# State product in 32-column tiles of the TensorE array, its PSUM banks moved next to the first-layer banks

## The reference

```python
# gated linear attention, 4 sequences of 768 tokens, 8 heads of 48
for t in range(S):
    state = alpha[:, :, t, :, None] * state + einsum('bhd,bhe->bhde', k[:, :, t], v[:, :, t])
    y[:, :, t] = einsum('bhd,bhde->bhe', q[:, :, t], state)
# four experts, 384 -> 1024 -> 384, weighted by normalised probabilities
h = np.maximum(x @ w1[e], 0.0);  out += p[:, e:e + 1] * (h @ w2[e])
# gated feed-forward, 384 -> 2048 -> 384
h = x @ w_in;  g = h * clip(h + 3, 0, 6) / 6;  out = g @ w_out
```

## Time and profile before

| | us |
|---|---|
| median of 3 runs | 1381.57 (1380.89 to 1384.29) |
| profiled execution, its own time | 1382.56 |
| span of the profiled execution, first to last instruction | 1380.6 |
| PE busy | 1356.1 (98%) |
| POOL, DVE, ACT busy | 790.9, 699.7, 534.8 |
| L438 matmuls (state product) | 704 records, 20.4 us busy |

### The profile page before, as it was taken

The page is one execution under the profiler, slowest core; times in us unless marked ns, Lnnn a source line. Parts: engine busy times, 40 slices in busy tenths (PEclk is TensorE's granted clock), DMA queues, the critical chain, the costliest instruction groups (busy, mean ns, idle before and its releaser), DMA issues.

```text
span 1380.6 us, 34120 instructions
## 1 busy us (share of the span) xinstructions
PE 1356.1 (98%) x13596; PEld 1105.3 (80%) x13596; DVE 699.7 (51%) x1401; ACT 534.8 (39%) x992; POOL 790.9 (57%) x863
## 2 busy tenths in 40 slices
PE   6799999999999999999999999999999999999998
PEld 5578888888888888888888888888888888888887
DVE  8877665444454554454544544454445443333333
ACT  2233334333354333354433344533335433335543
POOL 7877665656565656565656565656564444444442
PEclk7899999999999999999999999999999999999999
DMA  4243343343334433433443334343322343333331
GB/s 146 73 144 119 115 117 117 104 125 95 110 96 126 126 118 103 119 95 114 130 126 104 109 96 126 104 124 112 114 85 85 99 128 106 104 99 92 99 118 35
DMA packets 70667, 150.33 MB, mean 109 GB/s; under 512 B 9584, under 2 KB 22128, under 8 KB 70512
## 3 DMA queue, kind: packets, MB, share of 16 engines
q1 hardware_dynamic: 70512, 148.16, 35.8%
HBM read 143.36 MB, written 4.77 MB: 107 GB/s over the span
## 4 chain that ended last, share of the span: by engine, by line
PE 95%; issue 0%; DVE 0%; ACT 0%; DVEq 0%
PE psum L517 43%; PE psum L501 42%; PE psum L417 5%; PE psum L458 1%; PE psum L438 1%; PE psum L428 1%; PE psum L473 1%; PE psum L481 1%; DVE result L664 0%; DVE psum L644 0%; DVE x_lo L660 0%; ACT gate L779 0%; ACT x_hi L799 0%; DVEq L148 0%; ACT w_hi L792 0%
## 5 line engine op out<-in xcount | busy, mean ns | idle before, releaser
L892 POOL TENSOR_TENSOR w_lo<-w_raw,w_hi 128x768 fp32r<-128x768 f32 (+1 forms) x291 | 531.7, 1828 | 537.2 <-ACT w_hi L792 537.2
L786 ACT ACTIVATE h_hi<-psum 128x512 fp32r<-128x512 f32 x288 | 172.6, 599 | 628.1 <-DVE psum L638 553.3
L517 PE MATMUL psum<-h_hi,w_hi 128*128 128x512 f32 x864 | 344.8, 399 | 0.2 <-DVE x_lo L660 0.2
L517 PE MATMUL psum<-h_hi,w_lo 128*128 128x512 f32 x864 | 337.3, 390 | 0.0
L501 PE MATMUL psum<-x_hi,w_hi 128*128 128x512 f32 x864 | 336.5, 389 | 0.3 <-issue 0.3
L517 PE MATMUL psum<-h_lo,w_hi 128*128 128x512 f32 x864 | 336.7, 390 | 0.0
L501 PE MATMUL psum<-x_lo,w_hi 128*128 128x512 f32 x864 | 336.1, 389 | 0.0
L501 PE MATMUL psum<-x_hi,w_lo 128*128 128x512 f32 x864 | 336.1, 389 | 0.0
L638 DVE SCALAR_TENSOR_TENSOR psum<-psum,probs 128x512 f32<-128x512 f32 x192 | 134.2, 699 | 349.4 <-PE psum L501 349.3
L792 ACT ACTIVATE w_hi<-w_raw 128x768 fp32r<-128x768 f32 x288 | 241.4, 838 | 0.0
L650 DVE TENSOR_TENSOR h_lo<-psum,h_hi 128x512 fp32r<-128x512 f32 x288 | 197.3, 685 | 46.5 <-ACT h_hi L786 46.5
(11 more groups left out here) (52 smaller groups left out, 717.4 us busy)
## 6 DMA issues: line engine op xcount, KB each, us to landing
w_raw<-w SPq DMA_DIRECT2D x288, 384.0 KB, 3.1
alpha_q<-qa SPq DMA_DIRECT2D x48, 256.0 KB, 3.8
k_raw<-kk SPq DMA_DIRECT2D x48, 128.0 KB, 3.7
probs<-prob_scratch SPq DMA_DIRECT2D x24, 256.0 KB, 3.6
v_diag<-v SPq DMA_DIRECT2D x96, 48.0 KB, 2.5
out<-result SPq DMA_DIRECT2D x18, 256.0 KB, 4.0
level_sb<-level SPq DMA_DIRECT2D x1, 80.0 KB, 3.2
ident_sb<-ident SPq DMA_DIRECT2D x1, 64.0 KB, 2.9
```

Of the source, the lines that this page charges most:

```text
L517: mm = pe.matmul(out_bank[k], a, x[:, g % DEEP, :], start=first and i == 0, stop=last and i == 2)
L786: act.activation(h_hi[:, g % DEEP, :], h_bank[g % 2][:, :], ACT.Copy).then_inc(hh_made, 1)
L892: op = pool.tensor_tensor(w_lo[:, g % RING, cols], w_raw[:, g % RAW, cols], w_hi[:, g % RING, cols].bitcast(F32), ALU.subtract)
```

## The change

`carry(n)` is done in `64*32` tiles: 16 matmuls (32 records) in place of 8 (16 records), each with half of the array columns, ordered so that eight neighbouring matmuls go to eight different tiles. Its results lie in other PSUM banks. The banks are laid out anew: 0 and 2 are the `h_bank`s, 1 holds the transposed keys, 3 and 4 the scores, 5 to 7 the second layer's output. The state product uses bank 1 and beside it the `h_bank` that the current slot does not use: `spare(n)` is 0 or 1, and the pair is banks `spare(n)` and `spare(n) + 1`. Two waits keep this safe. Ahead of `carry(n)`, from chunk 8 on, PE waits until `hidden_lo(g - 1)` is done (`hl_made` at `state_slot(n)`). Ahead of `hidden(g + 1)` it waits for `s_made`, that is, until `next_state(n)` has read the product. `keep_warm` writes to bank 7.

```diff
--- before.py
+++ after.py
@@ -185,11 +185,11 @@
         copied = sb("copied", [P, 1])
 
         psum = ctx.enter_context(nc.psum_tensor("psum", [P, 8 * BANK], F32))
-        state_bank = psum[:, 0:BANK]
-        score_banks = psum[:, BANK:3 * BANK]
-        out_banks = psum[:, 3 * BANK:5 * BANK]
-        out_bank = [psum[:, i * BANK:(i + 1) * BANK] for i in (3, 4, 5)]
-        h_bank = [psum[:, i * BANK:(i + 1) * BANK] for i in (6, 7)]
+        state_bank = psum[:, BANK:2 * BANK]
+        h_bank = [psum[:, i * BANK:(i + 1) * BANK] for i in (0, 2)]
+        score_banks = psum[:, 3 * BANK:5 * BANK]
+        out_banks = psum[:, 5 * BANK:7 * BANK]
+        out_bank = [psum[:, i * BANK:(i + 1) * BANK] for i in (5, 6, 7)]
         kt_out = state_bank[:, 0:2 * P]
 
         in_qa = [sem(f"in_qa{i}") for i in range(QRING)]
@@ -252,14 +252,17 @@
 
             return out_banks if n < PER_TILE and n % 2 else score_banks
 
+        def spare(n):
+
+            return n % 2 if n < PER_TILE else (state_slot(n) + 1) % 2
+
         def kv_bank(n, jj):
 
-            return scores(n)[:, BANK:2 * BANK] if jj else state_bank
+            return psum[:, (spare(n) + jj) * BANK:(spare(n) + jj + 1) * BANK]
 
         def kv_out(n):
 
-            stride = (4 if n < PER_TILE and n % 2 else 2) * BANK
-            return psum[:, 0:2 * stride].rearrange("p (a c) -> p a c", a=2)[:, :, KV_AT:KV_AT + 2 * HEAD_D].rearrange(
+            return psum[:, spare(n) * BANK:(spare(n) + 2) * BANK].rearrange("p (a c) -> p a c", a=2)[:, :, KV_AT:KV_AT + 2 * HEAD_D].rearrange(
                 "p a (b e) -> p b a e", b=2)
 
         def y_rows(n):
@@ -431,13 +434,16 @@
 
             def carry(n):
 
+                if n >= PER_TILE:
+                    pe.wait_ge(hl_made, state_slot(n))
                 for jp in range(2):
-                    for i in range(2):
-                        for jj in range(2):
-                            lo = KV_AT + jp * HEAD_D
-                            mm = pe.matmul(kv_bank(n, jj)[own(i), lo:lo + HEAD_D], k_rows[own(jj), jp, own(i)],
-                                           v_diag[n % 2][own(jj), jj, jp, i, :], start=jp == 0 and jj == 0, stop=True,
-                                           skip_group_check=True)
+                    for jj in range(2):
+                        for i in range(2):
+                            for d in range(2):
+                                lo, rows = KV_AT + jp * HEAD_D, quarter(i, d)
+                                mm = pe.matmul(kv_bank(n, jj)[rows, lo:lo + HEAD_D], k_rows[own(jj), jp, rows],
+                                               v_diag[n % 2][own(jj), jj, jp, i, :], start=jp == 0, stop=True,
+                                               skip_group_check=True)
                 return mm
 
             def attend(n):
@@ -478,7 +484,7 @@
 
             def keep_warm(n):
                 for _ in range(n):
-                    pe.matmul(h_bank[0][:, 0:2 * P], zeros_sb[:, 0:P], zeros_sb[:, :], start=True, stop=True)
+                    pe.matmul(out_bank[2][:, 0:2 * P], zeros_sb[:, 0:P], zeros_sb[:, :], start=True, stop=True)
 
             def hidden(g):
 
@@ -492,6 +498,8 @@
                     pe.wait_ge(out_free, K3 * (PHASES.index(("E", t)) + 1))
                 need(pe, hh_made, g - 1)
                 need(pe, hl_made, g - 1)
+                if g - 1 in STATE_AT and not last_of_seq(STATE_AT[g - 1]):
+                    pe.wait_ge(s_made, carried(STATE_AT[g - 1]) + 1)
                 pe.wait_ge(w_hi_made, g + 1)
                 pe.wait_ge(w_lo_made, g + 1)
                 for k in range(K3):
```

## The result

The changed kernel takes 1387.99 us (median of 5 runs, 1387.48 to 1389.34) against 1382.52 us (5 runs, 1380.89 to 1384.29) for the kernel before: ratio 1.0040, 95% interval 1.0028 to 1.0051, so about 5.5 us slower. That is 0.5 us inside the upper end of the range given and 6.2 us over the forecast, on the slower side of 0.3%, while the likeliest case was no difference. The profiled execution took 1387.68 us (span 1385.9).

What follows compares the result with a forecast made beforehand. PE, holding 95% of the chain, was taken as the bound: 1382.56 - 4.4 (attends) + 4.4 (waits) - 0.3 (first stage) = 1382.3, or 1381.3 against the median; between them 1381.8 us was named, range 1377 to 1388.5.

Steps and rivals of the forecast that it cites:

- The first new wait: State product waits for the low hidden part at chunks 8, 10, 13: PE later by 2.79, 0.81, 0.82 us, 4.4 in all.
- The floor of 0.58 us: In an attend, L473 can't start sooner than 0.58 us after L458, as read in chunk 23, which has no state product.
- The gain of an attend: From chunk 8 on: 0.13 us less per ordinary attend, 0.17 at three sequence starts; 4.4 us without the three waiting attends.
- PE can't be fed: Rival, attends: supply of 96 records sets the pace, +0.21 us in 30 attends, +7.0 us, so 1393 us; chance 0.14.
- The change of tile kind costs 0.13 us: Between blocks of an attend: the missing 0.13 us behind L458 and behind L473 is what changing the tile kind costs.
- The second new wait at nothing: Ahead of the next hidden product, PE's wait for the state to be made is covered by second-layer work; costed at nothing.
- The first stage: Eight chunks where DVE and POOL set the pace: PE gains at most 1.5 us, of which 0.3 was taken.
- instruction reading as luck of either sign: Rival, first stage: PE's unexplained 2.74 us idle time can vanish (1379) or come twice (1384.7); chance 0.08.
- The half clock behind the stall: Rival, chunk 8: after 2.8 us idle the clock halves for 6.8 us, +2.5 us, 1384.3; chance 0.23.
- half-strength feed case: Slow supply of PE's records at half strength; with a half clock and bad luck it set the range's upper end, 1388.5.

Runs made afterwards that it cites:

- The deal of 2 and 5: The changed kernel with VectorE's query steps dealt 2 and 5, not 4 and 3, over the two slots behind a score slot: 1384.18 us, ratio 1.0011.
- the doubled L458: The kernel before, with the product of kept scores and v done twice in a row from chunk 8 on, old banks, no new wait: 1397.39 us (one run).

## Why the prediction was right or wrong

- **The first new wait: right.** Three places and no other; forecast 2.79, 0.81 and 0.82 us later, measured 2.7, 0.9 and 0.9 on the first-layer starts (4.4 us of waiting, as summed). The deal of 2 and 5 shows the cause: with fewer query steps ahead of the subtraction 3.6 of the 4.4 us of waiting go. (I had allowed 0.15 us from DVE's end to PE's start, it was 0.06.)
- **The floor of 0.58 us: met, but not as a floor.** L479 starts there. "This is robust", I wrote, and so it was as far as L479's start. But the waits of PE name L464 for L479 only at four places, the last chunks of sequences. In an ordinary attend the product's own records go on to 0.60 us and the first of L479 start among them, so the pace alone would have put L479 there. That the two numbers agree is luck.
- **The gain of an attend: wrong, and the step that failed** is "with no change of kind, it starts 0.21 us after L458 and takes 0.21", with its silent sequel that L473 would keep its 0.33. Measured: 0.25, 0.33 and 0.45, 1.03 in all. The pace of 6.5 ns was read from a block of 32 that stands behind long matmuls, and used for 96 in a row. The attend won 0.01 us where I wrote 0.13, and a slot with one 0.05 through its long products; the attends of the first chunks of a sequence grew by 0.02 to 0.07 and won no 0.17. In sum 1.6 us for 4.4. This is the rival "PE can't be fed" in a weak form: it holds in kind, but the attend stayed just under its old 1.04 us, so its +7 us did not come. The Trainium skill bears on the size ("TensorE: Matmul & The Clock Gate", table at its head: TensorE has a queue of 64 instructions): 32 records with their weight loads are 64. No run here looks into the queue itself, but a store of that size fits the rows.
- **The change of tile kind costs 0.13 us: fits.** From the last record of a block to the first of another kind it is 0.13 us in chunk 17 before, and also behind a slow block (chunk 24 after, the doubled L458). Without a change of kind, L464 to L444 is 0.25 in place of 0.33, a difference of 0.08 only, because the fast pace ends there.
- **The second new wait at nothing: right.** No wait for `state` ahead of the first layer in any profile.
- **The first stage: wrong in sign.** I took 0.3 us off; it ended 2.3 us later in this profile, 1 to 2 in the others. I had named instruction reading as luck of either sign with a chance of 0.08 (its "come twice" should read 1384.5, not 1384.7), and had not counted that 32 more records, weight loads among them, in each of eight chunks also load PE there. PE works at half clock for much of the stage: 44 us of it in this profile and 31 before. By the table above both the records and the clock have a part; what the clock follows is open. One such stretch, which answers to the earlier trace rows:

```profile
45.50:55.70 10.20, 9.27 (x253) 7.38 (x254) 8.62 (x22) 2.83 (x12) 7.97 (x18) 0.50 0.30 70
```

- **The half clock behind the stall** had 0.23 and came in five of seven profiles. It lasts 3.4 us and costs 1.6 us, not 2.5. The two profiles compared in the account above have none of it.

The sum by the measured terms: 4.5 for the waits, 2.3 for the first stage, less 1.6 for the attends: +5.2 us for the profile without the half clock, where the forecast's terms gave -0.3 (4.4, less 0.3, less 4.4). The miss is the gain of the attends, 2.8 us too high, and the first stage, 2.6 us too low, in about equal parts. That the time still lies in the range is in part luck: its upper end was drawn for a half clock and a half-strength feed case, and the first stage, which made near half of the miss, was in it only as an idle time that comes twice.

## What to carry to other kernels

A pace read from a block of small matmuls holds for a block of that length behind long work. If a change puts such blocks in a row or doubles one, look for the pace of the 33rd record, not of the first 32. A bank that is borrowed from another pipeline brings that pipeline's slowest step as a wait: look up how late the lender's last reader is at every place, since three of 36 places made 4.4 us of waiting here, and a table entry of the reader's engine took most of it back.

## What the runs showed of the hardware

The records of `64*32` fp32 matmuls start 6.5 ns apart for 32 records and about 8 to 11 ns apart after that, in any bank and order that was tried, and 6.5 again after an idle time or three long matmuls. From a block's last start to the first start of a block of another tile kind it is 0.13 us. Unexplained idle times of 0.3 to 4.2 us inside PE's blocks of the first stage stood at one record in 256, always the same count, in all 13 profiles. Behind an idle time of 2.75 us within dense work the half clock came for 3.4 us in five of seven profiles; in the one profile in which dummy matmuls filled it, none came.
